# SyncE's list of transfers in a chunked recurrence reordered, and the first two triangular solves given out anew

## The chip, the core and the metric

The kernel runs on one core of a Trainium2 chip. TensorE multiplies matrices, VectorE and GpSimd (POOL) work on tiles in the on-chip memory, ScalarE copies and scales, and SyncE (SP) issues the DMA transfers, one after the other in program order. Engines meet through semaphores: an engine that comes to a wait holds up everything behind it on its own list. The metric is the time of one execution in microseconds; lower is better.

## The reference, cut to what matters

A linear recurrence runs over 768 tokens for 4 x 8 heads with a 40 x 40 state each; its output then goes through a gated feed-forward layer and a four-expert attention layer. The change touches only the recurrence:

```python
for t in range(S):
    y[:, :, t] = np.einsum('bhd,bhde->bhe', rt, state)
    Sa = np.einsum('bhde,bhe->bhd', state, at)
    state_decay = state * wt[:, :, None, :] - np.einsum('bhd,bhe->bhde', Sa, bt)
    state = state_decay + np.einsum('bhd,bhe->bhde', vt, kt)
```

## The kernel before, in words

**Tiles and steps.** The tokens are cut into 12 chunks of 64, the 32 heads into two groups, which gives 24 tiles. Every engine has its own list and walks over steps n = -6 to 24. Step n finishes tile n on TensorE and ScalarE, and prepares later tiles: VectorE makes the decay products of tile n+6 (`prefixes`, L296, `suffixes`, L302, `bk`, L310, and last in its step `al`, L317, which raises `prepped`), TensorE multiplies tile n+5 (`g_products`, L102), and VectorE masks the result into `ak_and_l` (`gm`, L326). I call the moment at which this masking begins in step n gm(n).

**The solve.** Within a chunk the tokens depend on each other through a unit triangular matrix. Two tiles, 2j and 2j+1, form pair j (12 pairs). Their blocks are written to DRAM by SP (`l_out`, L463, four transfers per tile), read back with one block per partition into `l_by_unit` (`l_in`, L474, two transfers), and inverted there column by column: 31 columns, two dependent instructions each, a product (L285) and a subtraction (L287). VectorE does the first 9 columns (`solve_head(j)`, 18 instructions, in step 2j-3, between its `suffixes` and its `gm`), POOL the other 22 (44 instructions, the tail). Then SP writes the inverse out (`t_out(j)`, L482) and reads it back (`t_in`, L492), in step 2j-1; TensorE needs it in step 2j (`first_blocks`, L131). `prefixes` and `gm` are one tile each; a head stands in every second, odd step.

**SP's list in a step** before the change: on odd steps from -1 `t_out` and `t_in`; `l_out(n+5)`; `load_x(n+8)` (L440, six transfers of 642 KB in all, which wait for `prepped` of tile n+6); `load_v(n+2)` (L446); `l_in(n+5)`; `load_r(n+2)` (L452, L453); now and then a `store`. The v and r of the first two tiles stand at its very start. `load_x` has two buffers, `l_in` must wait until `l_out` of the same tile has landed. ScalarE's copy of the other half of that product (`bkn_move`, L238) waits for `gm` and stands in its list ahead of the copy that TensorE's second solve product (L173) needs, so a late `gm` holds TensorE too.

## Time and profile before

| what | value |
|---|---|
| median of 3 runs | 1002.92 us (1001.4 to 1010.96) |
| the profiled execution | 1008.42 us, span 1006.5 us |
| busy: PE, DVE, ACT, POOL | 824.0, 546.5, 311.3, 265.0 us |
| recurrence with solves under way | to about 404 us |
| mean granted TensorE clock | 0.936 |

Times in the trace are counted from the start of the span. The profiled execution is one run; it lies 5.5 us above the median. About the last 570 us are the feed-forward and attention layers, whose code the change leaves as it is.

### The profile page before, as it was taken

The page shows a single profiled execution, that of the slowest core. Times are in us where ns is not written, and L with a number is a line of the kernel's source. Part 1 is how long each engine was busy: PE and PEld are TensorE (multiplying, and loading weights), DVE is VectorE, ACT ScalarE, POOL GpSimd, SP SyncE. Part 2 cuts the span into 40 slices and gives each one's busy share as a digit, 9 for nine tenths or more (in the row PEclk, how much of TensorE's full clock was granted, in tenths as well). Part 3 has the DMA queues.
Part 4 walks back from the last instruction along what each step waited for, and adds up shares of the span by engine and source line. Part 5 has one row for each costly group of instructions (what it writes and reads, how often), then busy time and mean ns, then how long its engine had stood idle before and what let it go on. Part 6 is the DMA issues. An engine that isn't in the chain of part 4 may idle for free.

```text
span 1006.5 us, 27784 instructions
## 1 busy us (share of the span) xinstructions
PE 824.0 (82%) x11872; PEld 602.0 (60%) x11872; DVE 546.5 (54%) x1209; ACT 311.3 (31%) x739; POOL 265.0 (26%) x550
## 2 busy tenths in 40 slices
PE   2328989797789988759998789998899987899977
PEld 2228888796789878754454554455544545554555
DVE  7765675566667754124445635437454366353464
ACT  3002231132222322112225532225422255312354
POOL 1287876386667876000000000000000000000000
PEclk9998985787878989789999999999999999999999
DMA  5326556455655646323010000100000000000000
GB/s 138 98 66 126 134 123 135 83 129 113 124 125 136 131 89 146 70 75 106 1 40 8 20 14 1 40 0 21 14 7 16 24 8 20 14 1 0 1 21 20
DMA packets 133305, 61.33 MB, mean 61 GB/s; under 512 B 107328, under 2 KB 120256, under 8 KB 133184
## 3 DMA queue, kind: packets, MB, share of 16 engines
q1 hardware_dynamic: 133184, 59.56, 25.0%
q8 instruction: 94, 1.54, 0.7%
q14 instruction: 27, 0.22, 0.1%
HBM read 45.37 MB, written 14.16 MB: 59 GB/s over the span
## 4 chain that ended last, share of the span: by engine, by line
PE 57%; DVE 15%; SPq 7%; ACT 6%; DMA 6%; issue 5%; POOL 5%; DVEq 0%; ACTq 0%
PE ps_all L715 9%; PE ps_all L699 8%; PE ps_all L756 4%; DMA l_by_unit<-l_blocks 4%; PE ps_all L832 3%; PE ps_all L793 3%; ACT probs L892 3%; SPq L440 3%; PE ps_all L811 3%; PE ps_all L709 3%; PE ps_all L823 2%; POOL t_update L285 2%; PE ps_all L702 2%; POOL t_by_unit L287 2%; PE ps_all L743 2%
## 5 line engine op out<-in xcount | busy, mean ns | idle before, releaser
L285 POOL TENSOR_TENSOR t_update<-l_by_unit,t_by_unit 128x126 f32<-128x126 f32 (+17 forms) x264 | 126.8, 480 | 118.6 <-DVE t_by_unit L287 98.7
L287 POOL TENSOR_TENSOR t_by_unit<-t_by_unit,t_update 128x126 f32<-128x126 f32 (+17 forms) x264 | 132.7, 503 | 20.7
L699 PE MATMUL ps_all<-scaled_then_x,inputs_then_w_up 128*128 128x384 f32 x256 | 90.9, 499 | 14.9 <-DMA scaled_then_x<-y_t 9.2
L102 PE MATMUL ps_scan<-decayed_a_and_eye,scaled_then_x 40*128 40x104 f32 x768 | 67.9, 346 | 38.1 <-DVE decayed_a_and_eye L317 38.1
L983 DVE TENSOR_REDUCE minus_max<-ps_all 128x1 f32<-128x128 f32 (+5 forms) x96 | 55.0, 617 | 75.4 <-PE ps_all L797 75.3
L715 PE MATMUL ps_all<-gated,w_down 128*128 128x384 f32 x256 | 91.1, 499 | 0.0
L102 PEld LDWEIGHTS ps_scan<-decayed_a_and_eye,scaled_then_x 40*128 40x128 f32 x768 | 62.9, 252 | 40.1 <-DVE decayed_a_and_eye L317 24.3
L699 PEld LDWEIGHTS ps_all<-scaled_then_x,inputs_then_w_up 128*128 128x128 f32 x256 | 48.8, 194 | 51.4 <-issue 11.2
L858 ACT ACTIVATE h<-ps_all 128x384 f32<-128x384 f32 x64 | 27.9, 490 | 147.9 <-PE ps_all L702 147.9
L715 PEld LDWEIGHTS ps_all<-gated,w_down 128*128 128x128 f32 x256 | 46.0, 189 | 44.6 <-issue 19.1
L793 PE MATMUL ps_all<-k_t,q_t 64*128 64x512 f32 (+3 forms) x256 | 49.7, 488 | 26.0 <-ACT probs L892 22.2
L929 DVE TENSOR_SCALAR conv<-h,w_conv 128x768 f32<-128x768 f32 x32 | 19.8, 620 | 93.9 <-ACT h L858 93.9
L238 ACT ACTIVATE bk_natural<-ps_scan 128x320 f32<-128x320 f32 x48 | 21.0, 437 | 151.2 <-DVE ak_and_l L326 151.2
L903 ACT ACTIVATE probs_t<-ps_all 128x512 f32<-128x512 f32 (+3 forms) x128 | 54.1, 451 | 31.0 <-PE ps_all L811 31.0
L892 ACT ACTIVATE probs<-ps_all,minus_max 128x128 f32<-128x128 f32 (+5 forms) x96 | 61.1, 638 | 6.3 <-DVE minus_max L983 6.3
L811 PE MATMUL ps_all<-identity,probs 128*128 128x128 f32 x336 | 51.7, 282 | 11.7 <-ACT probs_t L903 7.6
L173 PE MATMUL ps_scan<-x_rhs,block_inverse_t 64*64 64x40 f32 x768 | 33.5, 254 | 33.5 <-ACT x_rhs L227 33.4
L332 DVE TENSOR_TENSOR uv_and_ruv<-ps_scan,mask_strict 128x512 f32<-128x512 f32 x48 | 30.9, 685 | 49.1 <-PE ps_scan L165 49.1
L173 PEld LDWEIGHTS ps_scan<-x_rhs,block_inverse_t 64*64 64x64 f32 x768 | 30.5, 164 | 39.1 <-ACT x_rhs L227 37.8
L811 PEld LDWEIGHTS ps_all<-identity,probs 128*128 128x128 f32 x336 | 37.9, 141 | 24.8 <-issue 11.0
L193 PE MATMUL ps_scan<-uv_and_ruv,bk_natural 128*40 128x104 f32 x768 | 50.6, 299 | 0.6 <-DVE uv_and_ruv L332 0.6
L976 DVE TENSOR_SCALAR probs<-probs,inv_row_sum,expert_weight 128x128 f32<-128x128 f32 (+5 forms) x96 | 49.2, 512 | 3.5
(115 smaller groups left out, 1523.0 us busy)
## 6 DMA issues: line engine op xcount, KB each, us to landing
inputs_then_w_up<-in_x SPq DMA_DIRECT2D x48, 160.0 KB
l_by_unit<-l_blocks SPq DMA_DIRECT2D x48, 128.0 KB, 3.7
inputs_then_w_up<-in_x SPq DMA_DIRECT2D x48, 81.4 KB
inputs_then_w_up<-in_x SPq DMA_DIRECT2D x48, 80.0 KB
uv_and_ruv<-in_v SPq DMA_DIRECT2D x48, 80.0 KB, 4.2
r_t<-in_r SPq DMA_DIRECT2D x48, 80.0 KB
v_t<-in_vt SPq DMA_DIRECT2D x48, 80.0 KB
y_t<-y_out SPq DMA_DIRECT2D x24, 160.0 KB
```

The lines of the kernel that those rows point to most:

```text
L102: last = nc.tensor.matmul(PS[:, o:o + ROWS], weights, AL[c % NK][rows(h), p, :], start=True, stop=True)
L173: last = nc.tensor.matmul(PY[own(q), seg(p, D)], DT[n % 3][own(q), p, :], ZS[own(q), p, :], start=True, stop=True)
L193: last = nc.tensor.matmul(PS[rows(h), o:o + ROWS], BKN[n % NK][:, h, p, :], UV[n % 3][:, h, p, :], start=False, stop=True, skip_group_chec ...
L285: return (lambda: eng.tensor_tensor(tmp[:, 0:cols, 0:rest], l[:, s:s + 1, s + 1:BLK].broadcast_to(shape), t[:, 0:cols, s:s + 1].broadcast_ ...
L287: lambda: eng.tensor_tensor(t[:, 0:cols, s + 1:BLK], t[:, 0:cols, s + 1:BLK], tmp[:, 0:cols, 0:rest], ALU.subtract))
L699: nc.tensor.matmul(bank[n][:, 0:HALF], WIN[:, t, cols], XT[:, t, n * HALF:(n + 1) * HALF], start=(t == 0), stop=False)
L715: i = nc.tensor.matmul(down(t, n), WOUT[:, g, t * 128:(t + 1) * 128], GT[g % 3][:, n * HALF:(n + 1) * HALF], start=(g == 0), stop=ends)
L793: nc.tensor.matmul(PS[:, o[e] + k0:o[e] + k1], QQ[e * HD:(e + 1) * HD, pair, qt * 128:(qt + 1) * 128], KK[e * HD:(e + 1) * HD, pair, k0:k1 ...
L811: i = nc.tensor.transpose(bank[4 + n % 2][:, (k - k0) * 128:(k - k0 + 1) * 128], PR[v % NPR][:, k * 128:(k + 1) * 128], ID[:, :])
L892: nc.scalar.activation(PR[v % NPR][:, 0:n], PS[:, first_bank(v) * 512:first_bank(v) * 512 + n], ACT.Exp, bias=NM[:, v:v + 1], scale=-1.0, ...
L903: nc.scalar.activation(PTS[w % 2][:, k0:k1, v % 2, :], bank[4 + n % 2][:, 0:(k1 - k0) * 128].rearrange("p (k q) -> p k q", q=128), ACT.Cop ...
L983: nc.vector.tensor_reduce(NM[:, v:v + 1], PS[:, first_bank(v) * 512:first_bank(v) * 512 + n], AX.X, ALU.min).then_inc(m["nm"], 1)
```

## The change

SP: `load_x` is issued one step later but as the first thing of it; `l_in` follows `l_out` of its tile directly; `load_v` and `load_r` come behind both; the first v and r move from step -6 to step -4. VectorE: pair 0 is solved whole, all 31 columns, in step -2 behind `gm`; it has no part in pair 1. POOL: no part in pair 0; it solves pair 1 whole, from its own wait on `l_in`; pairs 2 to 11 are shared as before. Semaphore counts follow.

```diff
+        def solve_first():
+            for x in range(2):
+                dve.wait_ge(m[f"l_in{x}"], 32)
+            dve.wait_ge(m["eye"], 1)
+            for s in range(BLK - 1):
+                mult, sub = step(nc.vector, LU[0], TS[0], TMD, s)
+                link(dve, mult())
+                if s < BLK - 2:
+                    link(dve, sub())
+                else:
+                    sub().then_inc(m["solved"], 1)
...
-            if n % 2 == 1 and 0 <= (n + GA - 3) // 2 < NPAIR: solve_head((n + GA - 3) // 2)
+            if n % 2 == 1 and 2 <= (n + GA - 3) // 2 < NPAIR: solve_head((n + GA - 3) // 2)
             if ahead: gm(g)
+            if n == -2: solve_first()
             if prep: bk(c)
...
-        for j in range(NPAIR):
-            pool.wait_ge(m["head"], j + 1)
-            if j >= 1:
+        for j in range(1, NPAIR):
+            if j == 1:
+                for x in range(2):
+                    pool.wait_ge(m[f"l_in{x}"], 64)
+                pool.wait_ge(m["eye"], 2)
+            else:
+                pool.wait_ge(m["head"], j - 1)
                 pool.wait_ge(m["solved"], j)
-            for s in range(HEAD, BLK - 1):
+            for s in range(0 if j == 1 else HEAD, BLK - 1):
...
-            if n == -GA:
+            if n == 2 - GA:
                 for k in range(2):
                     load_v(k)
                     load_r(k)
+            if 2 <= n + GA + 1 < NT: load_x(n + GA + 1)
             if n >= -1 and n % 2 == 1 and n + 1 < NT:
                 t_out((n + 1) // 2)
                 for x in range(2): t_in(n + 1 + x)
-            if 0 <= c < NT: l_out(c)
-            if n + GA + 2 < NT: load_x(n + GA + 2)
-            if 0 <= n and n + 2 < NT: load_v(n + 2)
-            if 0 <= c < NT: l_in(c)
-            if 0 <= n and n + 2 < NT: load_r(n + 2)
+            if 0 <= c < NT:
+                l_out(c)
+                l_in(c)
+            if 0 <= n and n + 2 < NT:
+                load_v(n + 2)
+                load_r(n + 2)
```

**SP in an even step.** This is step 0 of SP's list before; later even steps read alike. A row is the line, the kind, the tile written and the tile read, and the shape.

```order
71 L463 DMA l_blocks<-ak_and_l 32x8x32 x4
72 L440 DMA inputs_then_w_up<-in_x 40x521
...
77 L440 DMA inputs_then_w_up<-in_x 40x512
78 L446 DMA uv_and_ruv<-in_v 64x8x40 x2
79 L474 DMA l_by_unit<-l_blocks 32x1024 x2
80 L452 DMA r_t<-in_r 40x512
```

And now, where every line number from L440 on is 20 higher:

```order
70 L460 DMA inputs_then_w_up<-in_x 40x512
71 L483 DMA l_blocks<-ak_and_l 32x8x32 x4
72 L494 DMA l_by_unit<-l_blocks 32x1024 x2
73 L466 DMA uv_and_ruv<-in_v 64x8x40 x2
74 L472 DMA r_t<-in_r 40x512
...
78 L460 DMA inputs_then_w_up<-in_x 40x521
```

The read-back of the blocks moves ahead of six x transfers and two v transfers; the x transfers now stand directly ahead of the next write of blocks.

**SP at the start.** Steps -6 to -4 before (the v and r of tiles 0 and 1 are rows 13 to 22 there, ahead of these):

```order
24 L440 DMA inputs_then_w_up<-in_x 40x1024
...
29 L463 DMA l_blocks<-ak_and_l 32x8x32 x4
30 L440 DMA inputs_then_w_up<-in_x 40x521
...
36 L474 DMA l_by_unit<-l_blocks 32x1024 x2
37 L463 DMA l_blocks<-ak_and_l 32x8x32 x4
38 L440 DMA inputs_then_w_up<-in_x 40x521
```

And now:

```order
19 L483 DMA l_blocks<-ak_and_l 32x8x32 x4
20 L494 DMA l_by_unit<-l_blocks 32x1024 x2
21 L466 DMA uv_and_ruv<-in_v 64x8x40 x2
...
30 L473 DMA v_t<-in_vt 40x512
31 L460 DMA inputs_then_w_up<-in_x 40x521
...
36 L460 DMA inputs_then_w_up<-in_x 40x512
37 L483 DMA l_blocks<-ak_and_l 32x8x32 x4
38 L494 DMA l_by_unit<-l_blocks 32x1024 x2
```

Ten rows of v and r now stand ahead of the x of tile 3 and of the write and read of tile 1's blocks.

**VectorE at the first solve.** Step -3 before, with the head of pair 0 between `suffixes` and `gm`:

```order
28 L302 SCALAR_TENSOR_TENSOR suffix_products<-inputs_then_w_up,reset_inverses 104x520
29 L285 TENSOR_TENSOR t_update_first<-l_by_unit,t_by_unit 128x31
...
46 L287 TENSOR_TENSOR t_by_unit<-t_by_unit,t_update_first 128x5x23
47 L326 TENSOR_TENSOR ak_and_l<-ps_scan,mask_strict 128x512 x2
```

And now steps -3 and -2:

```order
28 L302 SCALAR_TENSOR_TENSOR suffix_products<-inputs_then_w_up,reset_inverses 104x520
29 L326 TENSOR_TENSOR ak_and_l<-ps_scan,mask_strict 128x512 x2
...
35 L326 TENSOR_TENSOR ak_and_l<-ps_scan,mask_strict 128x512 x2
36 L285 TENSOR_TENSOR t_update_first<-l_by_unit,t_by_unit 128x31
...
97 L287 TENSOR_TENSOR t_by_unit<-t_by_unit,t_update_first 128x16
98 L310 TENSOR_TENSOR scaled_then_x<-inputs_then_w_up,suffix_products 104x1024
99 L317 TENSOR_TENSOR decayed_a_and_eye<-inputs_then_w_up,prefix_products 104x8x64
```

The solve moves one step later, behind two maskings, and grows from 18 to 62 instructions, with `bk` and `al` of tile 4 behind it.

## Rows read from the trace of the kernel before

**Rows 1.** Busy time by stage: eight pairs; of the eight even-to-odd stretches last and sum

```profile
core 0: us, PE busy (x) PEld busy (x) DVE busy (x) ACT busy (x) POOL busy (x), PEclk, DMA share, GB/s
98.90:357.20 258.30, 219.71 (x6168) 209.94 (x6164) 175.07 (x337) 66.54 (x152) 179.23 (x352) 0.82 0.56 123
...
340.80:357.20 16.40, 13.59 (x448) 12.78 (x444) 13.05 (x30) 4.38 (x10) 11.63 (x25) 1.00 0.59 141
sum 148.70, PE 123.91 PEld 117.22 DVE 103.68 ACT 35.01 POOL 83.91; mean PE 15.49 PEld 14.65 DVE 12.96 ACT 4.38 POOL 10.49
```

**Rows 2.** VectorE in order of time, steps 10 and 11: start, duration, work, idle before

```profile
247.64 1.29 DVE L326 TENSOR_TENSOR ak_and_l<-ps_scan,mask_strict 128x512 f32<-128x512 f32 x2 [2.08 <-PE ps_scan L102]
251.88 0.72 DVE L317 TENSOR_TENSOR decayed_a_and_eye<-inputs_then_w_up,prefix_products 104x512 f32<-104x512 f32 x1
255.73 1.24 DVE L302 TENSOR_TENSOR_SCAN suffix_products<-inputs_then_w_up,reset_inverses 104x520 f32<-104x520 f32 x1
260.94 0.19 DVE L285 TENSOR_TENSOR t_update_first<-l_by_unit,t_by_unit 128x31 f32<-128x31 f32 x1 [3.97 <-DMA l_by_unit<-l_blocks]
265.64 1.28 DVE L326 TENSOR_TENSOR ak_and_l<-ps_scan,mask_strict 128x512 f32<-128x512 f32 x2
```

**Rows 3.** SP's issues in the same stretch, and one `t_out` to `l_out` later on

```profile
248.95 2.99 SPq L463 DMA_DIRECT2D l_blocks<-ak_and_l  x4
252.63 2.18 SPq L440 DMA_DIRECT2D inputs_then_w_up<-in_x  x6
254.86 1.22 SPq L446 DMA_DIRECT2D uv_and_ruv<-in_v  x2
256.19 1.02 SPq L474 DMA_DIRECT2D l_by_unit<-l_blocks  x2
259.43 3.72 SPq L482 DMA_DIRECT2D t_blocks<-t_by_unit  x4
267.75 1.93 SPq L463 DMA_DIRECT2D l_blocks<-ak_and_l  x4
```

**Rows 4.** VectorE's head behind step 16, which has no `load_x`

```profile
352.32 0.19 DVE L285 TENSOR_TENSOR t_update_first<-l_by_unit,t_by_unit 128x31 f32<-128x31 f32 x1 [2.16 <-DMA l_by_unit<-l_blocks]
```

**Rows 5.** Issue to landing of L463 alone, then of all that touch `l_by_unit`

```profile
DMA to landing us min/median/max: 1.5/2.0/3.7
DMA to landing us min/median/max: 2.8/3.7/5.2
```

**Rows 6.** POOL in order of time: one tail's first and last

```profile
298.86 0.38 POOL L285 TENSOR_TENSOR t_update<-l_by_unit,t_by_unit 128x110 f32<-128x110 f32 x1 [6.98 <-DVE t_by_unit L287]
324.69 0.24 POOL L287 TENSOR_TENSOR t_by_unit<-t_by_unit,t_update 128x16 f32<-128x16 f32 x1
```

**Rows 7.** The start, SP and VectorE in order of time

```profile
8.32 1.31 SPq L446 DMA_DIRECT2D uv_and_ruv<-in_v  x2
...
15.45 0.33 SPq L453 DMA_DIRECT2D v_t<-in_vt  x1
24.14 1.24 DVE L296 TENSOR_TENSOR_SCAN prefix_products<-inputs_then_w_up,reset_ones 104x520 f32<-104x520 f32 x1 [2.46 <-DMA inputs_then_w_up<-in_x]
42.24 0.28 DVE L287 TENSOR_TENSOR t_by_unit<-t_by_unit,t_update_first 128x115 f32<-128x115 f32 x1
70.01 2.64 SPq L482 DMA_DIRECT2D t_blocks<-t_by_unit  x4
82.28 1.29 DVE L326 TENSOR_TENSOR ak_and_l<-ps_scan,mask_strict 128x512 f32<-128x512 f32 x2 [9.33 <-PE ps_scan L102]
98.85 1.28 DVE L326 TENSOR_TENSOR ak_and_l<-ps_scan,mask_strict 128x512 f32<-128x512 f32 x2
```

**Rows 8.** POOL beside a VectorE scan, POOL beside a head, and VectorE in that head

```profile
53.34 1.27 POOL L287 TENSOR_TENSOR t_by_unit<-t_by_unit,t_update 128x128 f32<-128x128 f32 x1
61.22 0.47 POOL L287 TENSOR_TENSOR t_by_unit<-t_by_unit,t_update 128x110 f32<-128x110 f32 x1
62.26 0.43 DVE L287 TENSOR_TENSOR t_by_unit<-t_by_unit,t_update_first 128x56 f32<-128x56 f32 x1
```

More of the change, by code:

```diff
@@ L353, in solve_head @@
             dve.wait_ge(m["eye"], j + 1)
-            if j >= 1:
-                dve.wait_ge(m["head"], j)
+            dve.wait_ge(m["solved"], 1)
+            if j >= 3:
+                dve.wait_ge(m["head"], j - 2)
             for s in range(HEAD):
@@ L415, in gpsimd @@
         i.then_inc(m["set_pool"], 1)
-        for j in range(NPAIR):
-            pool.wait_ge(m["head"], j + 1)
-            if j >= 1:
+        for j in range(1, NPAIR):
[5 more added lines that the diff above has]
+                pool.wait_ge(m["head"], j - 1)
                 pool.wait_ge(m["solved"], j)
-            for s in range(HEAD, BLK - 1):
+            for s in range(0 if j == 1 else HEAD, BLK - 1):
                 mult, sub = step(nc.gpsimd, LU[j % 2], TS[j % 2], TMP, s)
@@ L424, in gpsimd @@
                 pool.wait_ge(m["pool_chain"], done)
+                if s == BLK - 2:
+                    pool.wait_ge(m["solved"], j)
                 i = sub()
```

## Prediction, made before the changed kernel was run

> **What bounds the kernel now.** I read the stages first. Between gm(1) at 98.9 and gm(17) at 357.2 the recurrence does eight pairs of tiles in 258.3 us [rows 1], 32.3 us each, with no engine full: TensorE 219.7, VectorE 175.1, POOL 179.2 us busy. What comes behind, the last steps without solves and the two layers, runs code that is not edited. So the change can act at the start (before 98.9) and in these eight pairs.
>
> Next, VectorE's list in one pair. gm(10) starts at 247.64; VectorE is through with `suffixes` at 255.73 + 1.24 = 257.0, 9.3 us after it; then it stands until 260.94 for the blocks of the pair (3.97 us by the row), works 4.7 us on the head, and gm(11) starts at 265.64 [rows 2]. ScalarE and TensorE hang on gm(11), so this stand lies on the path. SP shows why the blocks are late: it writes them at 248.95, then comes to `load_x`, which waits for `al` (ends 252.6, [rows 2]) and starts at 252.63, then v, and only at 256.19 the read-back [rows 3]. The transfer before had long landed: a write takes 2.0 us in the median [rows 5]. The stretch from even gm to odd gm is 148.7 us over the eight pairs, 18.6 each [rows 1]; the other half, odd to even, is the remainder, 109.6 us or 13.7 each.
>
> The start is another matter. The first solve is the path: head until 42.5, POOL's tail until SP writes the result at 70.01 [rows 7], because tile 0 cannot begin without it.
>
> **The even stretch.** With `l_in` directly behind `l_out`, from an even gm: masking 1.3 [rows 2]; to the issue of the fourth write 1.45 (1.93 for four, [rows 3]); its landing 2.4 (median 2.0, longest 3.7 [rows 5]; I take a value nearer the median, since x is now issued directly ahead of it); the second read-back issued 0.6 later; its landing 3.8 (median 3.7, longest 5.2 [rows 5]). That is 9.6 us, against 9.3 at which VectorE is ready: the two meet, so more than this can't be had. The head then takes 4.7 us, plus about 0.8, since POOL's tail will still run under it (below), and 0.1 of handover: 15.2 instead of 18.6. Step 16 is a sample of it, as it has no `load_x`: the stretch took 16.4 us [rows 1], with a stand of 2.16 us before the head [rows 4].
>
> **What is late next.** Three rings now come within 1 us of each other. (a) Compute: 13.7 + 15.2 = 28.9 us a pair. (b) POOL and SP: a tail takes 298.86 to 324.93 = 26.1 us [rows 6]; then `t_out`, `t_in` until SP reaches `l_out` 8.3 (259.43 to 267.75, [rows 3]); write and landing 1.45 + 2.4; read-back issue 1.0; v and r 2.7 (1.2 of v by rows 3, and four more at 0.35); a `store` in half of the steps 0.4; `load_x` 2.2 [rows 3]; then the even write, landing, read-back as above without the masking, 8.3; head 5.5. Sum 26.1 + 8.3 + 3.85 + 1.0 + 2.7 + 0.4 + 2.2 + 8.3 + 5.5 = 58.4 over two pairs, 29.2 a pair. Before, `load_x` lay beside the landing of the writes; now SP stands there, which is how the reordering pays back a part. (c) SP's own list without any wait for an engine: 8.3 + 2 x (3.85 + 1.0 + 2.7 + 2.2 + 0.4) = 28.6. With three rings of nearly equal length the longest of each pair counts; I take **29.5**. Saved: 8 x (32.3 - 29.5) = **22.4 us**. Bounds: 28.2 a pair (every landing at its median, head 4.7) gives 33; 31.2 (landings half way to their longest) gives 9. The tail's end under the head is the price of 0.8: the tail begins at an odd gm and lasts 26.1, the next head begins after 13.7 + 9.6 = 23.3.
>
> **The start.** Gain first: without v and r at the front, x of tile 2 no longer comes late (2.46 us of stand at 24.14, [rows 7]); gm(-4) begins at 24.5 instead of 26.9. Then the loss: SP writes and reads tile 0's blocks until about 24.2 (my estimate: masked at 19.9, then 1.45 + 2.0 + 0.9), and the 12 transfers of v and r follow, which took 7.5 us before (8.32 to 15.78, [rows 7]), 6.3 if nothing backs up; x of tile 3 is issued from 30.5 on; its 642 KB need 5.2 us at the 123 GB/s of rows 1, with a landing some 36.6 (before, VectorE was held by no x after that of tile 2). From there VectorE: two products 2.8, masking 1.3, `bk` and `al` 1.9, then the same for tile 4, whose x lands about 44: gm(-2) from 46.7 to 48.0. Now `solve_first`: 62 instructions instead of 18. Alone an instruction takes 0.19 [rows 2] to 0.28 us [rows 7] by its size, 0.03 between, 17.7 us in all (18 of them 4.75, 44 at 0.294). Tile 3's blocks are written after 48.0 and back at about 56.3; there POOL starts on pair 1, and beside POOL a VectorE instruction has POOL's pace, 0.47 instead of 0.25 [rows 8]. By 56.3 VectorE has done 30 instructions; 32 at 0.43 are 13.9: pair 0 is solved at **70.2**, the same as before. But `bk` and `al` of tile 4 come behind it (2.0), SP's `load_x(6)` waits for that `al`, and `t_out(0)` stands behind these six issues (2.3): 74.5 instead of 70.0. That is 4.5 us late at tile 0. POOL is through with pair 1 at about 89 (56.3 + 26.1 + 18 instructions at 0.4), earlier than anyone asks. gm(0) then comes at 86.8 instead of 82.3, and the stretch to gm(1), 16.6 before [rows 7], takes 9.6 + 4.7 + 0.2 = 14.5: gm(1) at about 101.3 instead of 98.9. Cost of the start **2.5 us**. Bounds: -1 (x of tile 3 at once, solve alone) and +9.
>
> A rule speaks against this double solve. In rows 8 a POOL product takes 1.27 us beside a VectorE scan of 1.24, and 0.47 beside a head, where VectorE takes 0.43: there neither waits for the whole of the other. The Trainium skill ("SBUF — State Buffer", Who interferes with whom) says that a VectorE instruction with two SBUF inputs and a GpSimd one that reads SBUF exclude one another for the whole instruction. The 1.27 us beside the scan agrees; the head beside the tail does not, and I go by it. By the rule the case is the third rival.
>
> **Sum.** 22.4 - 2.5 = 19.9 us off the profiled 1008.4 gives 988.5; off the median of 1002.9, **983**.
>
> **Rivals.** (1) SP becomes the bound. Ring (b) at 31.2 us: 8 x 1.1 - 2.5 = 6 off, **997**. For it: SP gets 4 us a pair of standing at landings. Against: before, it issued the write at 248.95, right at the end of the masking at 248.93 [rows 2, 3], so it was standing there; its list has slack to give. (2) Slower: the transfers of one queue are served in order, and x (642 KB) now directly precedes the writes of an even step. At the 123 GB/s of this part [rows 1] x alone needs 5.2 us. If a write lands 5.2 us and the read-back its longest 5.2 us after issue, the stretch is 1.3 + 1.45 + 5.2 + 0.6 + 5.2 + 5.5 = 19.3, and x itself reaches `prefixes` late by about 1 us: 20.3, +1.7 x 8 + 2.5 = 16 more, **1019**. It decides from the point where both landings together pass 9.6 us; forecast 6.2. Against it: writes took 3.7 us at most [rows 5], over all 96 of them, some of which followed an x closely. (3) The exclusion: each of the 32 instructions costs its own 0.28 and POOL's 0.33 to 0.40, 20.5 us instead of 13.9; the start costs 9: **990**. (4) More: TensorE's granted clock is 0.82 of full in the eight pairs and 1.00 in the last even stretch [rows 1]; of the two levels, 1.2 and 2.4 GHz, the lower rules after long stands of TensorE behind a late gm. Shorter stands may keep it up: clock at 0.95 would shorten an odd stretch by 1.5 us, 8 x 1.5 = 12 more, POOL's ring permitting: **971**.
>
> **Chances.** Forecast (977 to 989) 0.52; SP bound 0.16; slower 0.11; exclusion 0.08; more 0.13. About 1% (10 us) is what a measurement of this kernel can tell from no change. Below 992.9: the forecast, rival 4, most of 3 and a little of 1: 0.72. Within 1%: most of 1, the rest of 3, a mild form of 2: 0.20. Slower: 0.08. The range leaves out the slower case and the tail of rival 4, and reaches from 968 to 1001.
>
> **What would show it.** Right: VectorE's stand before an even stretch's head falls from about 4 us to under 1.5; gm to gm of a pair 29 to 30 us; the first write of the inverse near 74 us, not 70; SP's waits for `ak_and_l` shrink and waits for POOL grow; x of tile 3 holds VectorE for some 6 us near 30 to 37. Wrong: if the write of blocks lands 4 us or more after its issue, or if SP reaches even writes later than gm is done by over 2 us. The prediction fails most likely in how the three rings combine, and second in the start, where each microsecond goes to the end undiminished.

## The result and the profile after

The changed kernel is slower: 1032.82 us in the median of four runs (1030.53 to 1036.46), beside 1006.94 for the kernel before (four runs, 1001.4 to 1028.9). The ratio is 1.0279 [1.0204, 1.0354]; the runs of one kernel that lie over 1.5% above its fastest are left out of ratios, which bears on two kernels below (the fill with the new solves, and the change with early v and r), for the kernel before ran from 992.29 to 1026.39 us beside them and eleven of its 17 runs fall out. The forecast was 983 us in a range of 968 to 1001.

The profiled execution has a span of 1030.8 us, 24.3 more than before. The maskings divide this: gm(1) came at 106.95 instead of 98.85 [rows 7], +8.1; the eight pairs from there to gm(17) took 277.1 us instead of 258.3 [rows 1], +18.8, or 34.6 a pair instead of 32.3; what follows gm(17) took 646.8 instead of 649.3, -2.5. Over all the profiles of this document that last part lies between 642.8 and 651.9, so a few microseconds of difference between single profiles are no finding by themselves.

The page of the kernel after, its span and the engines' shares of the chain that ended last:

```profile
span 1030.8 us, 27803 instructions
...
PE 54%; SPq 14%; DVE 13%; DMA 9%; ACT 6%; issue 5%; ACTq 0%; DVEq 0%
```

SP's issues are 14% of that chain, and no POOL stands in it; before, the same line reads SPq 7% and POOL 5%. The eight pairs by busy time, same columns as [rows 1]:

```profile
106.90:384.00 277.10, 233.69 (x6126) 222.54 (x6128) 174.26 (x337) 66.21 (x152) 170.24 (x352) 0.76 0.50 114
```

VectorE, ScalarE and POOL have the same counts and about the same busy time as before, spread over 18.8 us more. TensorE is busy longer because its granted clock fell from 0.82 to 0.76 of full (of the two levels, 1.2 and 2.4 GHz, more of the lower one). That is no cause of its own here: the next lines show that SP hardly waits for any engine in the pairs, so a slower one can't hold it. SP's waits in the whole run of before (line, what for: us in total, times, the longest):

```profile
SPq L463 <- DVE ak_and_l L326: 38.2, 12, 9.2
SPq L482 <- POOL t_by_unit L287: 27.8, 8, 13.5
SPq L440 <- DVE decayed_a_and_eye L317: 13.2, 13, 2.6
SPq L492 <- DMA t_blocks<-t_by_unit: 6.4, 12, 1.3
SPq L474 <- DMA l_blocks<-ak_and_l: 0.9, 1, 0.9
```

and of after, where the write and the read-back of blocks are L483 and L494, those of the inverse L502 and L512, and x is L460:

```profile
SPq L494 <- DMA l_blocks<-ak_and_l: 49.3, 24, 3.6
...
SPq L512 <- DMA t_blocks<-t_by_unit: 22.9, 12, 3.8
...
SPq L460 <- DVE decayed_a_and_eye L317: 17.8, 1, 17.8
...
SPq L483 <- DVE ak_and_l L326: 4.4, 4, 3.2
SPq L502 <- POOL t_by_unit L287: 3.7, 1, 3.7
```

Before, SP waited for engines, 79 us in all; after, it hardly does once the pairs have begun (the one long wait of L460 is at the start), and stands 72 us for its own transfers to land. An engine that no longer waits for the others is the one that they wait for. SP's list in one pair of after, in order of time (start, duration of the issues, work):

```profile
214.07 4.94 SPq L512 DMA_DIRECT2D block_inverse_t<-t_blocks  x8
219.05 3.18 SPq L483 DMA_DIRECT2D l_blocks<-ak_and_l  x4
223.44 0.78 SPq L494 DMA_DIRECT2D l_by_unit<-l_blocks  x2
224.26 1.25 SPq L466 DMA_DIRECT2D uv_and_ruv<-in_v  x2
...
228.10 3.37 SPq L460 DMA_DIRECT2D inputs_then_w_up<-in_x  x6
231.51 2.76 SPq L483 DMA_DIRECT2D l_blocks<-ak_and_l  x4
236.25 0.78 SPq L494 DMA_DIRECT2D l_by_unit<-l_blocks  x2
```

There is no gap here that is not a landing: from 219.05 to 236.25 one issue follows the other, but for 1.2 us behind the first write and 2.0 behind the second. VectorE in the same stretch (the last bracket is the idle time ahead and what ended it):

```profile
224.20 1.29 DVE L326 TENSOR_TENSOR ak_and_l<-ps_scan,mask_strict 128x512 f32<-128x512 f32 x2 [5.52 <-PE ps_scan L102]
230.01 0.68 DVE L317 TENSOR_TENSOR decayed_a_and_eye<-inputs_then_w_up,prefix_products 104x512 f32<-104x512 f32 x1
235.55 1.24 DVE L296 TENSOR_TENSOR_SCAN prefix_products<-inputs_then_w_up,reset_ones 104x520 f32<-104x520 f32 x1 [4.87 <-DMA inputs_then_w_up<-in_x]
244.25 1.28 DVE L326 TENSOR_TENSOR ak_and_l<-ps_scan,mask_strict 128x512 f32<-128x512 f32 x2
```

gm(8) ended at 225.49, but SP came to its write only at 231.51, 6.0 us later. Before, the write of such a step was issued right behind the masking [rows 2, 3]. x is late too: `prefixes` waited 4.87 us for it. VectorE's longest waits for transfers in the eight pairs, before and then after:

```profile
DVE t_update_first L285 <- DMA l_by_unit<-l_blocks: 31.3, 8, 5.4
DVE prefix_products L296 <- DMA inputs_then_w_up<-in_x: 56.5, 8, 10.5
```

The stand ahead of the head, which the change was to remove, is gone: after the change no head waited for its blocks. But in every pair VectorE now stands for x, 7.1 us in the mean, which it never did here before. The even writes begin 1.4 to 11.1 us behind their maskings, 7.0 in the mean. The stretch from gm(8) to gm(9) took 20.05 us; over the eight pairs the even stretches sum to 170.2 us, 21.3 each, against 148.7 [rows 1]. The odd ones took 13.4 each, 13.7 before. So the loss in the pairs is all in the even stretches, where the change was to gain, and what VectorE stands for in them is x.

The same pair in the chain that ended last (start, duration, what; a DMA is its landing):

```profile
208.16 5.89 DMA t_blocks<-t_by_unit
...
221.78 1.64 DMA l_blocks<-ak_and_l
...
228.10 0.94 SPq L460
...
231.14 4.39 DMA inputs_then_w_up<-in_x
235.55 1.25 DVE prefix_products L296
...
244.25 1.29 DVE ak_and_l L326 x2
```

The chain leads through SP's whole list, x included, and only then to VectorE. To size this I summed the issue durations of SP's rows in the eight pairs, and the idle time ahead of each row by what ended it:

| us in eight pairs | before | after |
|---|---|---|
| length | 258.3 | 277.1 |
| issuing | 205.5 | 218.5 |
| idle ahead of rows that wait for an engine (gm 18.7, `al` 12.9, POOL 10.2) | 41.8 | 1.8 |
| idle ahead of the read-back of blocks | 1.8 | 33.8 |
| idle ahead of the read-back of an inverse | 4.8 | 19.0 |

(393 and 394 of some 400 transfers have a record; a missing one counts as idle, so the sums hold to a few us.) SP was already issuing for 80% of the stretch before. The new order took away 40 us of waits for engines, put 46 us of landings in their place, and issues for 13 us longer. So of the 18.8 us lost, about 6 are standing beyond the old slack and 13 are longer issues.

The start of after, VectorE and SP together in order of time:

```profile
37.12 1.24 DVE L296 TENSOR_TENSOR_SCAN prefix_products<-inputs_then_w_up,reset_ones 104x520 f32<-104x520 f32 x1 [8.55 <-DMA inputs_then_w_up<-in_x]
47.79 1.29 DVE L326 TENSOR_TENSOR ak_and_l<-ps_scan,mask_strict 128x512 f32<-128x512 f32 x2
70.64 0.19 DVE L287 TENSOR_TENSOR t_by_unit<-t_by_unit,t_update_first 128x16 f32<-128x16 f32 x1
73.08 2.78 SPq L460 DMA_DIRECT2D inputs_then_w_up<-in_x  x6
75.91 2.65 SPq L502 DMA_DIRECT2D t_blocks<-t_by_unit  x4
79.62 4.73 SPq L512 DMA_DIRECT2D block_inverse_t<-t_blocks  x8
89.77 1.29 DVE L326 TENSOR_TENSOR ak_and_l<-ps_scan,mask_strict 128x512 f32<-128x512 f32 x2 [6.65 <-PE ps_scan L102]
106.95 1.28 DVE L326 TENSOR_TENSOR ak_and_l<-ps_scan,mask_strict 128x512 f32<-128x512 f32 x2
```

VectorE has pair 0 solved at 70.83, but SP issues six x transfers first and writes the inverse at 75.91.

### The profile page after: what moved, and what is told of

Same layout as the page of the kernel before. It is cut to its first block, busy times and chain, and to the rows that moved or that the text cites. A ratio compares the mean times of both kernels' runs of the same rounds, so it can differ in the third digit from the quotient of the medians.

```text
span 1030.8 us, 27803 instructions
## 1 busy us (share of the span) xinstructions
PE 840.0 (81%) x11872; PEld 615.3 (60%) x11872; DVE 554.9 (54%) x1235; ACT 310.8 (30%) x739; POOL 239.4 (23%) x524
## 4 chain that ended last, share of the span: by engine, by line
PE 54%; SPq 14%; DVE 13%; DMA 9%; ACT 6%; issue 5%; ACTq 0%; DVEq 0%
PE ps_all L737 9%; PE ps_all L721 7%; PE ps_all L778 4%; SPq L460 4%; PE ps_all L815 3%; PE ps_all L854 3%; DMA l_blocks<-ak_and_l 3%; PE ps_all L833 3%; ACT probs L914 3%; DMA t_blocks<-t_by_unit 3%; PE ps_all L731 3%; PE ps_all L845 2%; PE ps_all L724 2%; SPq L512 2%; PE ps_all L765 2%
## 5 line engine op out<-in xcount | busy, mean ns | idle before, releaser
L285 POOL TENSOR_TENSOR t_update<-l_by_unit,t_by_unit 128x133 f32<-128x133 f32 (+13 forms) x251 | 116.8, 465 | 172.7 <-DVE t_by_unit L287 102.1
L102 PE MATMUL ps_scan<-decayed_a_and_eye,scaled_then_x 40*128 40x104 f32 x768 | 74.4, 369 | 83.1 <-DVE decayed_a_and_eye L317 58.1
L287 POOL TENSOR_TENSOR t_by_unit<-t_by_unit,t_update 128x133 f32<-128x133 f32 (+13 forms) x251 | 117.1, 467 | 19.7
L102 PEld LDWEIGHTS ps_scan<-decayed_a_and_eye,scaled_then_x 40*128 40x128 f32 x768 | 69.1, 274 | 85.4 <-DVE decayed_a_and_eye L317 44.4
L737 PEld LDWEIGHTS ps_all<-gated,w_down 128*128 128x128 f32 x256 | 46.0, 189 | 44.6 <-issue 19.1
L296 DVE TENSOR_TENSOR_SCAN prefix_products<-inputs_then_w_up,reset_ones 104x520 f32<-104x520 f32 x24 | 30.6, 1274 | 70.7 <-DMA inputs_then_w_up<-in_x 69.5
L925 ACT ACTIVATE probs_t<-ps_all 128x512 f32<-128x512 f32 (+3 forms) x128 | 54.1, 451 | 32.1 <-PE ps_all L833 32.1
L193 PE MATMUL ps_scan<-uv_and_ruv,bk_natural 128*40 128x104 f32 x768 | 55.4, 318 | 0.6 <-DVE uv_and_ruv L332 0.6
L833 PEld LDWEIGHTS ps_all<-identity,probs 128*128 128x128 f32 x336 | 38.2, 142 | 24.6 <-issue 11.4
L326 DVE TENSOR_TENSOR ak_and_l<-ps_scan,mask_strict 128x512 f32<-128x512 f32 x48 | 30.9, 685 | 35.8 <-PE ps_scan L102 31.9
L193 PEld LDWEIGHTS ps_scan<-uv_and_ruv,bk_natural 128*40 128x40 f32 x768 | 48.6, 151 | 2.4 <-issue 0.8
```

The lines of the kernel that those rows point to most:

```text
L102: last = nc.tensor.matmul(PS[:, o:o + ROWS], weights, AL[c % NK][rows(h), p, :], start=True, stop=True)
L193: last = nc.tensor.matmul(PS[rows(h), o:o + ROWS], BKN[n % NK][:, h, p, :], UV[n % 3][:, h, p, :], start=False, stop=True, skip_group_chec ...
L285: return (lambda: eng.tensor_tensor(tmp[:, 0:cols, 0:rest], l[:, s:s + 1, s + 1:BLK].broadcast_to(shape), t[:, 0:cols, s:s + 1].broadcast_ ...
L287: lambda: eng.tensor_tensor(t[:, 0:cols, s + 1:BLK], t[:, 0:cols, s + 1:BLK], tmp[:, 0:cols, 0:rest], ALU.subtract))
L737: i = nc.tensor.matmul(down(t, n), WOUT[:, g, t * 128:(t + 1) * 128], GT[g % 3][:, n * HALF:(n + 1) * HALF], start=(g == 0), stop=ends)
L833: i = nc.tensor.transpose(bank[4 + n % 2][:, (k - k0) * 128:(k - k0 + 1) * 128], PR[v % NPR][:, k * 128:(k + 1) * 128], ID[:, :])
```

## Experiments

The theory (A): SP's own list bounds the pairs; the issues take about 26 to 27 us a pair in any order, and the new order stands at landings with nothing to do. Rival (B): the solves given out anew, or the later v and r, cost the pairs. Rival (C): it is the bytes of x directly ahead of the short transfers, and not the length of the list. Two kernels were executed once, with the profile; the others are medians with their ratio to runs of the kernel before on the same chip.

**The three parts alone.** Each is put alone into the kernel before. SP's order alone, with v and r of the first two tiles at the front and the old solves:

```diff
+            if 2 <= n + GA + 1 < NT: load_x(n + GA + 1)
             if n >= -1 and n % 2 == 1 and n + 1 < NT:
...
-            if 0 <= c < NT: l_out(c)
-            if n + GA + 2 < NT: load_x(n + GA + 2)
-            if 0 <= n and n + 2 < NT: load_v(n + 2)
-            if 0 <= c < NT: l_in(c)
-            if 0 <= n and n + 2 < NT: load_r(n + 2)
+            if 0 <= c < NT:
+                l_out(c)
+                l_in(c)
+            if 0 <= n and n + 2 < NT:
+                load_v(n + 2)
+                load_r(n + 2)
```

> SyncE's new order in steps -5 to 24 alone; v and r of tiles 0 and 1 stay at its very start, the solves are shared out as before. Theory A (SP's list is what bounds the eight pairs: it stands at the landing of transfers queued right behind x): the pairs stay near 34.6 us as in the changed kernel instead of 32.3, so 8 x 2.3 = 18 us of the 27 us are here; with a start much as before, ratio about 1.018. Theory B (the pairs are longer because the new start shifts POOL's tails against VectorE): pairs at 32 us or less and a ratio of 0.98 to 1.00.

Measured: 1025.63 us, ratio 1.0229 [1.0151, 1.0307]. gm(1) at 96.9, the eight pairs 279.4 us. SP's waits:

```profile
SPq L474 <- DMA l_blocks<-ak_and_l: 56.5, 24, 4.9
...
SPq L482 <- POOL t_by_unit L287: 16.8, 3, 13.4
...
SPq L463 <- DVE ak_and_l L326: 10.7, 5, 5.9
```

The order alone gives the whole loss of the pairs (+21.1; the full change +18.8), and costs nothing at the start; the read-back of blocks again heads SP's waits. As in the changed kernel, VectorE stands for x, 62 us in the eight pairs. The solves alone:

```diff
+        def solve_first():
+            for x in range(2):
+                dve.wait_ge(m[f"l_in{x}"], 32)
+            dve.wait_ge(m["eye"], 1)
+            for s in range(BLK - 1):
+                mult, sub = step(nc.vector, LU[0], TS[0], TMD, s)
...
+            if n == -2: solve_first()
```

> The new sharing of the first two solves alone; SyncE's list as before, in full. Theory A: only the start moves. gm(-2) comes some 9 us earlier without a head ahead of it, the solve on VectorE takes 18 to 22 us against 32 us for head and tail, so tile 0 starts about 5 us earlier and the pairs keep 32.3 us: ratio 0.990 to 1.000. Theory B: pairs grow to 34 us or more, ratio 1.015 or more.

Measured: 1011.56 us, ratio 1.0103 [1.0027, 1.0179]. gm(0) at 78.39, earlier than the 82.28 of [rows 7], and gm(1) at 97.7 instead of 98.85; the eight pairs 260.0 us. SP and POOL around tile 3's blocks:

```profile
61.09 2.18 SPq L460 DMA_DIRECT2D inputs_then_w_up<-in_x  x6
63.77 0.78 SPq L494 DMA_DIRECT2D l_by_unit<-l_blocks  x2
68.35 1.03 POOL L285 TENSOR_TENSOR t_update<-l_by_unit,t_by_unit 128x31 f32<-128x31 f32 x1 [62.74 <-DMA l_by_unit<-l_blocks]
```

In the old order the read-back of tile 3 stands behind an x that waits for the `al` behind the long solve, so POOL began pair 1 at 68 (57 in the changed kernel) and was still at it when head 2 ran. So the solves save nearly 4 us to gm(0), keep 1.1 of it at gm(1), and change the pairs by +1.7. The ratio, above the 0.990 to 1.000 expected, says 1% slower, while the profiled spans differ by 1.1 us only; where the rest lies was not found. The later v and r alone:

```diff
-            if n == -GA:
+            if n == 2 - GA:
```

> Only the v and r of tiles 0 and 1 move from step -6 to step -4 of SyncE's list; all else as before. Both theories: the 12 transfers, 6 us, stand ahead of the write of tile 1's blocks, which the first head waits for, less the 2.5 us that x of tile 2 gains: the start about 3 to 6 us later, pairs unchanged, ratio 1.003 to 1.006.

Measured: 1014.36 us, ratio 1.0136 [1.0047, 1.0225]. gm(1) at 102.5 (+3.6), the eight pairs 261.5 us (+3.2, which I can't explain). The ratio is above the 1.003 to 1.006 expected. B is out for the pairs: neither part costs them more than 3.2 us, and SP's order costs 21.1.

**Other work in the landing.** If A is right, the order should gain once the landing of the write is filled with issues that are needed anyway. In the kernel before, v and r go between `l_out` and `l_in`, and x goes last:

```diff
             if 0 <= c < NT: l_out(c)
-            if n + GA + 2 < NT: load_x(n + GA + 2)
-            if 0 <= n and n + 2 < NT: load_v(n + 2)
+            if 0 <= n and n + 2 < NT:
+                load_v(n + 2)
+                load_r(n + 2)
             if 0 <= c < NT: l_in(c)
-            if 0 <= n and n + 2 < NT: load_r(n + 2)
+            if n + GA + 2 < NT: load_x(n + GA + 2)
```

> Before, with one other order in SyncE's steps: block write, then v and r of tile n+2, then the read-back, then x of tile n+8. v and r are issued while the write lands, so SP doesn't stand there, and x still comes behind the read-back. Theory A in its form that the standing counts (SP's list too long): SP's pair is shorter by two landings of 2 us or more and by what stands before them, the pairs fall to 29.5 to 31 us, ratio 0.976 to 0.990. Theory A in its form that x directly ahead of t_out and of the block write is the whole cost: x is still directly ahead of both, pairs near 33 to 34 us, ratio 1.005 to 1.015.

Measured: 996.64 us over ten runs, ratio 0.9917 [0.9884, 0.9949]; gm(1) at 100.0, the eight pairs 247.6 us, 30.95 each. SP's waits:

```profile
SPq L482 <- POOL t_by_unit L287: 31.2, 9, 13.7
SPq L463 <- DVE ak_and_l L326: 23.7, 10, 7.0
...
SPq L492 <- DMA t_blocks<-t_by_unit: 11.2, 12, 2.5
SPq L474 <- DMA l_blocks<-ak_and_l: 10.6, 5, 3.2
```

SP waits for engines again, and the eight pairs are 10.7 us shorter than before, 31.8 shorter than with the new order in the same surroundings. The issues themselves took 214.7 us in them, 214.4 in the new order: what differs is the standing, 1.9 us for blocks and 8.6 for inverses against 43.7 and 15.4. This pair of kernels is the cleanest test of A: x at the end of a step stands in the same place as x at the head of the next, directly ahead of the writes in both, so but for a `store` only v and r have moved. VectorE's stand for blocks is 12.4 us here instead of 31.3, that for x 5.8. The ratio just misses the 0.976 to 0.990 that was expected. The same order with the new solves:

```diff
-            if 2 <= n + GA + 1 < NT: load_x(n + GA + 1)
...
-            if 0 <= c < NT:
-                l_out(c)
-                l_in(c)
+            if 0 <= c < NT: l_out(c)
             if 0 <= n and n + 2 < NT:
                 load_v(n + 2)
                 load_r(n + 2)
+            if 0 <= c < NT: l_in(c)
+            if n + GA + 2 < NT: load_x(n + GA + 2)
```

> The order of e4_fill (block write, v and r, read-back, x) in all steps together with the new sharing of the first two solves; v and r of tiles 0 and 1 at step -6. The pairs should be those of e4_fill, 31 us, by every theory. The start: with the read-back ahead of x, POOL can begin pair 1 near 50 us and not at 68 as in e2_solves, so gm(1) should come 2 to 5 us earlier than the 100.0 of e4_fill: ratio 0.985 to 0.990, the fastest so far. If the solves only pay with the changed kernel's order, gm(1) stays at 99 to 100, ratio 0.991.

Measured: 995.38 us over twelve runs; gm(1) at 101.4, the eight pairs 247.3 us. The ratio is 0.9981 [0.9938, 1.0023], though the median of the kernel before beside it is 1009.69. The pairs repeat those of the run ahead (247.3 and 247.6 us); whether the kernel beats before is not settled by this run. At the start the expectation failed: gm(1) came 1.4 us later than without the new solves, not 2 to 5 earlier. Here, too, SP comes to the first inverse only behind an x that waits for the `al` behind the whole solve (x at 67.69, the inverse at 70.24).

**The start.** The changed kernel with the first v and r back at the front:

```diff
-            if n == 2 - GA:
+            if n == -GA:
```

> The changed kernel with v and r of tiles 0 and 1 back at step -6. If the late v and r are what makes its start dear (x of tile 3 stands behind them, and the whole solve behind that tile), gm(-2) comes near 40 us instead of 47.8, tile 0 some 7 us earlier, gm(1) near 99 to 100 instead of 107, and the pairs stay at 34.6 us: ratio near 1.020. If the start is dear through the solves themselves, gm(1) stays at 105 or more.

Measured: 1025.36 us, ratio 1.0287 [1.0214, 1.036]; gm(-2) at 43.1 instead of 47.8, gm(1) at 101.9 instead of 106.95, the eight pairs 273.8. SP ahead of tile 0:

```profile
68.17 2.51 SPq L460 DMA_DIRECT2D inputs_then_w_up<-in_x  x6
70.72 2.65 SPq L502 DMA_DIRECT2D t_blocks<-t_by_unit  x4
```

By the profiles the later v and r are worth 5.1 of the 8.1 us that the start lost, and 3.3 in the pairs, as in their own run; the ratio, though, is that of the change itself, where 1.020 was expected, so the gain is not shown in the time. The x ahead of the first inverse is still there: beside SP's order alone (gm(1) at 96.9) the new solves cost 5.0 us.

**Bytes or issues.** The changed kernel, in which the six transfers of x bring only their first 16 columns from tile 8 on. It leaves out most of the input of those tiles, so its output is not that of the reference:

```diff
-                    sp.dma_start(INX[c % 2][rows(h), lo:hi], in_x[c, h][:, lo:hi]).then_inc(m[f"inx{c % 2}"], 16)
+                    end = hi if c < 8 else lo + 16
+                    sp.dma_start(INX[c % 2][rows(h), lo:end], in_x[c, h][:, lo:end]).then_inc(m[f"inx{c % 2}"], 16)
```

> The changed kernel, but of x from tile 8 on only the first 16 columns of each of the six transfers are loaded, so its decay products and all that follow them are of other data; SyncE's list has the same transfers, in the same order and number. Theory A1 (bytes: x stands in the queue directly ahead of the transfers whose landing SP and VectorE wait for): with next to no bytes the landings go back to 2 us, x lands 2 us after issue, and the pairs from step 3 on fall from 34.6 us to 28 to 30. Theory A2 (SP's list with its standing is simply too long): issues and standing stay, pairs at 32 to 34.

Measured in one execution: 1012.88 us; gm(1) at 106.8, the eight pairs 252.4 us. SP's waits:

```profile
SPq L495 <- DMA l_blocks<-ak_and_l: 46.6, 24, 3.0
...
SPq L513 <- DMA t_blocks<-t_by_unit: 6.4, 12, 1.5
```

Without its bytes a pair is 3.1 us shorter, 24.7 in eight. A write of blocks lands in 2.0 us in the median (2.6 in the changed kernel), an inverse in 2.2 (3.6). The standing for inverses falls from 19.0 to 2.4 us, that for blocks only from 33.8 to 32.6; the other 7 us are issues, but not those of x, which take as long as in the changed kernel, 44.4 us in the eight pairs against 43.1. SP waits for no engine in these pairs, so its list is still the bound. The other half of the question, the same list but shorter: v and r of tile n+2 are issued by ScalarE:

```diff
+            if 0 <= n and n + 2 < NT:
+                k = n + 2
+                if k >= 3:
+                    act.wait_ge(m["out"], k - 2)
+                for h in range(2):
+                    act.dma_start(UV[k % 3][own(h), h, :, 0:D], in_v[k, h]).then_inc(m[f"v{k % 3}"], 16)
...
-            if 0 <= n and n + 2 < NT:
-                load_v(n + 2)
-                load_r(n + 2)
```

> The changed kernel, but v and r of tile n+2 are issued by ScalarE at the end of its step n, not by SyncE: the same bytes, a list on SP that is shorter by about 2 x 3 us a pair. Theory A2: the pairs fall by 4 to 6 us to 29 to 31, as SP no longer bounds them. Theory A1: the landings stay long behind x and, with the same bytes in fewer microseconds, the pairs stay at 33 us or more.

Measured in one execution: 1006.84 us; gm(1) at 107.0, the eight pairs 253.0 us. SP's waits:

```profile
SPq L503 <- DMA l_blocks<-ak_and_l: 47.3, 24, 3.4
SPq L492 <- DVE ak_and_l L335: 32.1, 11, 7.9
```

All bytes are there and the landings are as long as in the changed kernel, yet a pair is 3.0 us shorter, and SP waits for maskings again, 32.1 us. So C is half right: bytes and issues count, each 3 us a pair when it is taken away alone, by one execution each. Both lie between what the two theories had forecast for them.

**x in the landing of the inverse.** A filling for the other landing: in odd steps x goes between `t_out` and `t_in`. Into the kernel with early v and r (the changed one otherwise):

```diff
+            solved = n >= -1 and n % 2 == 1 and n + 1 < NT
+            if solved: t_out((n + 1) // 2)
             if 2 <= n + GA + 1 < NT: load_x(n + GA + 1)
-            if n >= -1 and n % 2 == 1 and n + 1 < NT:
-                t_out((n + 1) // 2)
+            if solved:
                 for x in range(2): t_in(n + 1 + x)
```

> e5_vr_early (the changed kernel with v and r of tiles 0 and 1 first) with one move: in odd steps x is issued between t_out and t_in, not ahead of t_out. SP stood 20.6 us in the eight pairs of the changed kernel before t_in, and the write of the inverse took 3.6 us to land behind x. List theory: this standing is filled by six issues, the pairs fall by 2 to 2.5 us from 34.2 to about 32, and t_out(0) goes out at 68 and not 70.7, so gm(1) is near 99: 20 us less than e5_vr_early, ratio 1.000 to 1.010. If the standing before t_in was covered, the pairs stay at 34.

Measured: 1009.16 us over ten runs, ratio 1.0027 [0.999, 1.0063]; gm(1) at 98.3, the eight pairs 258.6 us, 15.2 less than without this edit. The first inverse:

```profile
65.42 2.96 SPq L502 DMA_DIRECT2D t_blocks<-t_by_unit  x4
```

It is written 5.3 us earlier (70.72 without the edit) and gm(1) gains 3.6: this was the rest of the loss at the start. Standing for inverses fell from 16.1 to 0.9 us in the eight pairs, for blocks it rose from 34.4 to 41.6. Then on top of the kernel that fills the landing of the blocks, with the old solves, the x of an even step moves into the next odd step, between `t_out` and `t_in`:

```diff
+            solved = n >= -1 and n % 2 == 1 and n + 1 < NT
+            if solved: t_out((n + 1) // 2)
+            if n > 1 - GA and n % 2 == 1 and n + GA + 1 < NT: load_x(n + GA + 1)
...
-            if n + GA + 2 < NT: load_x(n + GA + 2)
+            if (n == -GA or n % 2 == 1) and n + GA + 2 < NT: load_x(n + GA + 2)
```

> e4_fill with the x that an even step issued moved into the next odd step, between t_out and t_in; solves as before. In e4_fill SP stands only 8.6 us before t_in and waits for POOL and the masking besides, so it no longer bounds: pairs from 30.95 us to 30.0 to 30.9, ratio 0.985 to 0.992. If SP's list still bounds e4_fill in part, pairs at 30 us or less.

Measured: 1002.38 us over twelve runs, ratio 0.9931 [0.9897, 0.9964]; gm(1) at 99.8, the eight pairs 252.1 us, 31.5 each, where 30 to 30.9 were expected. And with the new solves as well:

```diff
+        def solve_first():
...
+            if n == -2: solve_first()
```

> e10_fill_x_in_t with the new sharing of the first two solves. In e5_vr_early and e6_fill_solves t_out(0) stood behind an x that waits for the al after the whole solve (70.7 against 68.6 with the old solves in e1_sp_order); here it doesn't, so it should go out at 66 to 68 and gm(1) come at 97 to 99, 1 to 3 us ahead of e10_fill_x_in_t. If the new solves are no gain by themselves, gm(1) is at 100 or later and the two kernels take the same time.

Measured: 999.58 us over twelve runs, ratio 0.9898 [0.9864, 0.9932]; gm(1) at 98.1, the eight pairs 249.7 us. With both landings filled the pairs gain nothing more than with one: 1.9 us for blocks and 1.0 for inverses are left in the former of the two, and SP waits for engines, 32.0 us. The new solves are worth 1.7 us at gm(1) by these two profiles; the intervals of the two ratios overlap.

**A shorter list and a filled landing.** x in the landing of the inverse, v and r issued by ScalarE:

```diff
+                for h in range(2):
+                    act.dma_start(UV[k % 3][own(h), h, :, 0:D], in_v[k, h]).then_inc(m[f"v{k % 3}"], 16)
...
-                load_v(n + 2)
-                load_r(n + 2)
```

> e9_x_in_t with v and r of tile n+2 issued by ScalarE at the end of its step n, as in e8_vr_by_act. List theory: e9_x_in_t still has SP full (issues 221 and standing at landings 46 us in its 258.6), so taking some 50 us of v and r off its list must shorten the pairs from 32.3 to about 29 to 30.5 us, where VectorE, TensorE and POOL bound them, unless ScalarE's new issues delay its copies: ratio 0.975 to 0.992. If SP's list was not the bound any more in e9_x_in_t, the pairs stay at 32 us, ratio 1.00.

Measured: 1008.22 us over twelve runs, ratio 0.9968 [0.9931, 1.0004]; gm(1) at 98.4, the eight pairs 248.8 us, 31.1 each, where 29 to 30.5 were expected. SP issues for 167 us only and waits 44.6 us for engines. ScalarE pays for it; one of its issues and the copy behind it, in order of time:

```profile
198.81 2.01 ACTq L276 DMA_DIRECT2D uv_and_ruv<-in_v  x1
...
202.64 0.44 ACT L227 ACTIVATE x_rhs<-ps_scan 128x320 f32<-128x320 f32 x1 [3.83 <-issue]
```

The copy that TensorE's solve needs stood 3.83 us behind transfers being issued on its own engine.

| kernel | ratio to before | gm(1) | us a pair |
|---|---|---|---|
| before | 1 | 98.85 | 32.3 |
| the change | 1.0279 | 106.95 | 34.6 |
| its SP order alone | 1.0229 | 96.9 | 34.9 |
| its solves alone | 1.0103 | 97.7 | 32.5 |
| its late v, r alone | 1.0136 | 102.5 | 32.7 |
| the change, early v, r | 1.0287 | 101.9 | 34.2 |
| that, and x in the inverse's landing | 1.0027 | 98.3 | 32.3 |
| v, r in the blocks' landing | 0.9917 | 100.0 | 30.95 |
| that, with the new solves | 0.9981 | 101.4 | 30.9 |
| both landings filled | 0.9931 | 99.8 | 31.5 |
| both, with the new solves | 0.9898 | 98.1 | 31.2 |
| x in the inverse's landing, v, r by ScalarE | 0.9968 | 98.4 | 31.1 |

Three lie 0.7 to 1.0% below the kernel before, each interval below 1: v and r in the blocks' landing, both landings filled, and both with the new solves. Their intervals overlap, so none is the best. The other two with pairs near 31 us have intervals that reach over 1.

## Why the prediction was wrong

The sign was wrong, and the step that failed is ring (c), "SP's own list without any wait for an engine: [...] = 28.6". It took 34.6 us a pair. By its terms, from the sums of SP's rows:

| us a pair | forecast | measured |
|---|---|---|
| write the inverse, land, read it | 8.3 | 10.2 (2.8 + 2.4 + 5.0) |
| two writes of blocks with landings | 7.7 | 9.2 (5.0 + 4.2) |
| two read-backs | 2.0 | 1.9 |
| v and r of two tiles | 5.4 | 6.3 |
| x of two tiles | 4.4 | 5.4 |
| store and gaps | 0.8 | 1.6 |
| sum | 28.6 | 34.6 |

No term is far off, and nearly all are low, because each was read from one row and mostly from a short one. In the eight pairs of before four writes of blocks took 1.79 to 2.99 us, 2.35 in the mean, and the ring had 1.93; both are in [rows 3]. Six issues of x took 2.18 to 4.04, 2.44 in the mean, and the ring had 2.2. After, the means were 2.5 and 2.9. A check was at hand: SP's rows in the eight pairs of before sum to 205.5 us of issuing, 25.7 a pair, and my ring held only about 23.0 of issuing. With 25.7 and the forecast landings (5.6) the ring would have read 31.3, ahead of the other two and hardly below the 32.3 of before.

That ring would have meant a small gain. The rest of the miss is standing for an inverse, forecast 0.8 and measured 2.4 a pair, and the issues, which grew by 1.6 us a pair. Of the time to land the bytes of x right ahead make a part: with 16 columns of x an inverse lands in 2.2 us instead of 3.6, blocks in 2.0 instead of 2.6.

**Rivals.** Rival 1 had the mechanism, SP as the bound, and gave 31.2 us a pair and 997 us: the place was right, the size was not. The argument against it misread a row. That SP stood at 248.95 until the masking was done [rows 2, 3] showed 2.3 us a pair of slack (18.7 in eight), and all its slack was 41.8 us, less than the 46 us of new standing; I counted the slack at one row and never the sum. Rival 2 gave the right sign by another way: that both landings together pass 9.6 us. They took 2.6 + 2.4 us in the median; what was late was not the landing but the issue, 6.0 us behind the masking in the pair shown. Of rival 2 only its last clause came true, x late at `prefixes`, by 7.1 us a pair and not by 1. Rival 3, the exclusion: the whole solve ran from 49.00 to 70.83, forecast 48.0 to 70.2; its last 33 instructions, beside POOL, came every 0.41 us, near the 0.43 taken from the rows and far from the 0.64 of the exclusion. The Trainium skill ("SBUF — State Buffer", Who interferes with whom) has a VectorE instruction with two SBUF inputs and a GpSimd one that reads SBUF exclude one another; for these two chains this trace disagrees, as it did in [rows 8]: VectorE's instructions lasted 0.38 us in the mean and POOL's 0.36, one of VectorE's every 0.41 and one of POOL's every 0.44. (The POOL row of 1.27 us in [rows 8] is a subtraction, where I wrote of a product; nothing hangs on it.) Rival 4 went the other way: the clock fell to 0.76.

**The even stretch** was forecast at 15.2 us and took 21.3. It assumed that the write follows the masking at once and that VectorE stands for nothing else than the blocks. The write did come late, but no head waited for it; what the sum had at nothing is x at `prefixes`, 7.1 us a pair, late because SP's list was. The odd stretch (13.7) held: 13.4.

**The start** was right in its steps and short in its end. x of tile 3 held VectorE until 37.12 (36.6 forecast), gm(-2) 47.79 (46.7), solved 70.83 (70.2), POOL through with pair 1 at 90.86 (89), the inverse written at 75.91 (74.5), gm(0) 89.77 (86.8). Of the last miss 1.4 us was there at the write; the rest lies between write and gm(0), 13.9 us, where the kernel before took 12.3 [rows 7]. The stretch to gm(1) was 17.2 instead of 14.5. Neither the write (91.09, right behind the masking) nor the read-back was late there, and the head waited for nothing; VectorE itself was through with `suffixes` only 12.4 us after gm(0), having stood 2.1 us for x and 3.4 for TensorE, where I had taken the 9.3 of a later step. It was 11.1 already before. The cost was 8.1 instead of 2.5, within my bound of 9. By the profiles SP's order alone gains 2.0 at gm(1), the new solves on top of it cost 5.0, and the late v and r 5.1; 3.6 of the 5.0 go when the inverse is written ahead of x. So the new solves are no fixed gain at gm(1): 1.1 us in the old order and 1.7 with both landings filled, but a loss of 1.4 with one landing filled and of 5.0 in the new order.

**The signs I named.** VectorE's stand ahead of the head fell from about 4 us to nothing, as for a success, and the time grew all the same: the sign watched one wait, and the stand moved to x. SP's waits for `ak_and_l` did shrink, 38.2 to 4.4 us, but its waits for POOL did not grow; they fell from 27.8 to 3.7, which is how one tells the bound from its neighbour. The sign named for a failure, an even write over 2 us behind the masking, came.

**Open.** Six kernels with a changed list that waits for engines again end at 30.9 to 31.6 us a pair, none at the 28.9 of ring (a). Which of compute, POOL's ring and the clock holds them there was not separated. Nor is it known why the same transfers take 205.5 us to issue in the pairs of before and 218.5 after the change, which is 13 of the 18.8 us lost. That the list is full is not the reason by itself: with v and r in the blocks' landing SP waits 17 us for engines and still issues for 214.7. Nor is it known why v and r issued later at the start go with pairs that are longer by 3.2 and 3.3 us, each by one profile.

## What to carry to other kernels

Before a queue's order is changed, sum the issue time of its rows over the stretch and set it beside the stretch's length: at 80% issuing only the rest is slack, and what new standing and longer issues take beyond it is paid in full. A list priced from single rows comes out too short; take means. A write that is read back wants other issues between the two that wait for nothing: here nothing between them gave 34.9 us a pair, x, which waits for `al`, and v 32.3, and v and r 30.95. And when an engine's waits for all others vanish at once, it is the bound.

## What the runs showed of the hardware

- Issuing x costs by the transfer, not by the byte: its transfers took 43.1 us of SP in the eight pairs, and 44.4 with 16 columns each. Six issues in a row took 2.2 us in eight of 15 cases after the change and 3.4 to 4.6 in the other seven; before, three of 15 took over 2.4. What makes them longer was not found.
- Short transfers land later in a list where x goes directly ahead of them with all its bytes than with 16 columns: 2.6 instead of 2.0 us for blocks, 3.6 instead of 2.2 for an inverse, in the median; the longest landing of an inverse was 5.9. By my estimate from 123 GB/s the bytes of x take 5.2 us, part of which passes while x is still being issued.
- Transfers issued by ScalarE can hold its copies: 3.83 us ahead of one copy, 12.6 us ahead of three in all between 98 and 347 us, in a kernel whose SP had 44.6 us to spare.
- Two chains of instructions with both inputs in SBUF, one on VectorE and one on POOL, ran side by side at 0.41 and 0.44 us an instruction; alone, VectorE's first 29 of the same solve took 0.29 each.
